# Moved loads, stores and a constants' step in a fused attention and double MoE kernel

## The reference, cut to what matters

```
p_packed = sm_attn(p, k, v)              # 8 batches, 8 heads, 576 tokens, 32 packed rows, head_dim 64
x = sm_attn(q, p_packed, p_packed)       # softmax attention, both times
x = x as (batch, 576, 512)
xk, xr = mu * x + (1 - mu) * x_prev      # two mixes with the token before
k = relu(xk @ w_k) ** 2                  # 512 -> 1024
x = sigmoid(xr @ w_r) * (k @ w_v)        # first MoE part
h = x^T @ U @ V                          # over tokens, rank 32
u = x + h^T
out = u + relu(u @ w_ch1) @ w_ch2        # second MoE part, 512 -> 2048 -> 512
```

## Time and profile before

| | us |
|---|---|
| median of 3 runs | 1382.73 |
| lowest and highest | 1382.36, 1384.01 |
| the profiled execution | 1382.45 |
| its span in the trace | 1380.5 |
| PE busy in the span | 1321.9 |

### The profile page before, as it was taken

The page is one execution under the profiler, slowest core; times in us unless marked ns, Lnnn a source line. Parts: engine busy times, 40 slices in busy tenths (PEclk is TensorE's granted clock), DMA queues, the critical chain, the costliest instruction groups (busy, mean ns, idle before and its releaser), DMA issues.

```text
span 1380.5 us, 21487 instructions
## 1 busy us (share of the span) xinstructions
PE 1321.9 (96%) x7662; PEld 1133.7 (82%) x7662; DVE 958.7 (69%) x1559; ACT 701.4 (51%) x1232; POOL 209.4 (15%) x290
## 2 busy tenths in 40 slices
PE   6799999989998999989999999999999999999997
PEld 5677878878887888878999999888887888788885
DVE  3878878777877876675566765956568575866556
ACT  2456664555555466443545554645355444645352
POOL 5630112222121103422001100200011000200000
PEclk8899999999999999999999999999999999999999
DMA  9645465736465422983888899787666887578755
GB/s 223 146 85 83 130 125 141 149 103 130 123 139 133 99 49 80 282 247 100 261 252 265 249 270 320 238 238 216 199 222 182 260 227 213 182 206 210 219 191 128
DMA packets 439112, 252.50 MB, mean 183 GB/s; under 512 B 314496, under 2 KB 359584, under 8 KB 439008
## 3 DMA queue, kind: packets, MB, share of 16 engines
q1 hardware_dynamic: 432800, 239.25, 64.0%
q0 software_dynamic: 3824, 11.30, 2.7%
q10 hardware_dynamic: 2384, 0.59, 0.2%
HBM read 201.25 MB, written 49.81 MB: 182 GB/s over the span
## 4 chain that ended last, share of the span: by engine, by line
PE 51%; DVE 2%; DMA 1%; issue 1%; SPq 0%; ACT 0%; DVEq 0%; ACTq 0%
PE bank L1144 25%; PE bank L1230 23%; PE bank L887 1%; DMA w_ring<-w_parts 1%; PE bank L1041 1%; PE bank L873 1%; PE bank L852 1%; DVE u_parts L1105 0%; DVE acc L1278 0%; DVE hid_parts L1259 0%; DMA v_stage<-in_moe_V 0%; ACT hid_parts L1253 0%; SPq L1527 0%; DMA x_scratch<-x 0%; PE bank L969 0%
## 5 line engine op out<-in xcount | busy, mean ns | idle before, releaser
L1230 PE MATMUL bank<-hid_parts,w_ring 128*128 128x512 f32 (+1 forms) x1680 | 355.5, 369 | 4.9 <-issue 2.3
L1144 PE MATMUL bank<-u_parts,w_ring 128*128 128x512 f32 (+1 forms) x1680 | 354.0, 368 | 1.0 <-DVE hid_raw L1189 0.8
L1230 PEld LDWEIGHTS bank<-hid_parts,w_ring 128*128 128x128 f32 x1680 | 303.2, 188 | 55.6 <-issue 14.9
L1144 PEld LDWEIGHTS bank<-u_parts,w_ring 128*128 128x128 f32 x1680 | 304.8, 188 | 41.1 <-issue 1.3
L1253 ACT ACTIVATE hid_parts<-hid_raw 128x512 fp32r<-128x512 f32 (+1 forms) x280 | 164.9, 589 | 143.8 <-PE bank L1230 143.2
L1259 DVE TENSOR_TENSOR hid_parts<-hid_raw,hid_parts 128x512 fp32r<-128x512 f32 (+1 forms) x280 | 187.1, 674 | 64.1 <-ACT hid_parts L1253 60.7
L873 PE MATMUL bank<-xk_hi,wk_hi 128*128 128x384 f32 x384 | 132.7, 346 | 0.4 <-DVE x L947 0.4
L873 PE MATMUL bank<-xk_lo,wk_hi 128*128 128x384 f32 x384 | 129.5, 337 | 0.0
L873 PE MATMUL bank<-xk_hi,wk_lo 128*128 128x384 f32 x384 | 129.4, 337 | 0.0
L907 ACT ACTIVATE square<-bank 128x384 f32<-128x384 f32 x96 | 47.0, 489 | 143.9 <-PE bank L873 129.0
L887 PE MATMUL bank<-wv_hi,k_hi 128*128 128x512 f32 x288 | 113.6, 394 | 0.0
(11 more groups left out here) (171 smaller groups left out, 1921.6 us busy)
## 6 DMA issues: line engine op xcount, KB each, us to landing
w_ring<-w_parts SPq DMA_DIRECT2D x560, 256.0 KB, 3.6
w_parts<-early_out SPq DMA_DIRECT2D x21, 896.0 KB, 5.0
w_parts<-piece_out SPq DMA_DIRECT2D x11, 896.0 KB, 4.6
x_scratch<-x SPq DMA_DIRECT2D x144, 64.0 KB, 2.0
kq_parts<-in_k SPq DMA_DIRECT2D x112, 72.0 KB, 2.8
kq_parts<-in_q SPq DMA_DIRECT2D x112, 72.0 KB, 2.4
v_rows<-in_v SPq DMA_DIRECT2D x56, 128.0 KB
x_tiles<-x_scratch SPq DMA_DIRECT2D x6, 1024.0 KB, 6.6
```

The lines of the kernel that those rows point to most:

```text
L1144: last = nc.tensor.matmul(to, wring[:, e % RW, ct, a, :], uc[:, pos, b, ct, 0:w], start=(pos in FRESH and ct == 0 and a == 0 and b == 0), ...
L1230: last = nc.tensor.matmul(role(st, j, BANK_OF[pos])[:, 0:w], wring[:, e % RW, j, a, :], hid[:, no % RH, b, 0:w], start=(pos in FRESH and i ...
```

## The change

- `load_first_v` waits for the first pair of k's heads (`k0_in[0]`) and no longer for the first half of q; the weights' loads behind it still wait for that half.
- `omu` moves behind `norm1`, the last part of the second softmax of batch 0.
- `EARLY_AT` goes from (0, 6, 11, 17, 23, 33, 40) to (0, 5, 10, 15, 23, 30, 36).
- Some attention steps of the FIRST group move by a slot or two.
- The loads of V move from the last chunk to slot 12 of the LAST group, into the upper half of a buffer twice as wide; ACT's split of V also waits for the stores of the pieces of buffer 0. The u steps move one slot later.
- For the last pair, tiles 4 to 7 are stored half by SP and half by ACT.
- Idle turns: 112 for 96 behind `scores2`, 36 for 48 behind `outB`.

```diff
-EARLY, FIRST_AT, EARLY_AT = 18, (23, 31, 38, 45), (0, 6, 11, 17, 23, 33, 40)
+EARLY, FIRST_AT, EARLY_AT = 18, (23, 31, 38, 45), (0, 5, 10, 15, 23, 30, 36)
-IDLE_TURNS = {"first": 24, (0, "scores2"): 96, (0, "outB"): 48}
+IDLE_TURNS = {"first": 24, (0, "scores2"): 112, (0, "outB"): 36}
-        third = batch_slots(15, 17, 19, 20, 21, 22, 23, 25, 26, 28, 30, 34, 36)
-        fourth = batch_slots(37, 38, 40, 41, 42, 43, 44, 45, 47, 49, 50, 53, 55)
+        third = batch_slots(15, 17, 20, 22, 23, 24, 25, 26, 28, 29, 31, 34, 36)
+        fourth = batch_slots(37, 38, 40, 42, 43, 44, 45, 46, 47, 49, 50, 53, 55)
...
+            items += [("b_v_load",)] if s == 12 else []
...
-            items += {0: [("b_loads",)], 3: [("b_v",)], 4: [("u", 0, 0), ("u", 0, 1)], 5: [("u", 0, 2), ("u", 0, 3)],
-                      6: [("u", 0, 4), ("u", 0, 5)], 7: [("u", 0, 6), ("u", 0, 7)], 8: [("b_ring",)],
+            items += {0: [("b_loads",)], 3: [("b_v",)], 5: [("u", 0, 0), ("u", 0, 1)], 6: [("u", 0, 2), ("u", 0, 3)],
+                      7: [("u", 0, 4), ("u", 0, 5)], 8: [("u", 0, 6), ("u", 0, 7), ("b_ring",)],
...
         elif step == "pv":
-            items += [("load_v", 1), ("omu",)]
+            items.append(("load_v", 1))
+        elif step == "norm1":
+            items.append(("omu",))
...
-        v_stage = sb("v_stage", [P, S], scope=early)[:, :]
+        v_stage = sb("v_stage", [P, 2 * S], scope=early)[:, S:2 * S]
...
+    def store_out(eng, p, k, quads=None):
+        nt, half = sum_place(*TILES[k])
+        lo, w = tokens(p, half)
+        eng.wait_ge(turn_ok, len(TILES) * p + k + 1)
+        for quad in quads or (range(2) if shared_out(p, k) else range(4)):
...
+    def shared_out(p, k):
+        return p == NB - 1 and k >= 4
...
+                load_x2(0, 1)
+            elif item[0] == "b_v_load":
+                sp.wait_ge(att.x_act, 2 * B)
+                sp.wait_ge(att.x_dve, 2 * B)
                 for i in range(4):
                     sp.dma_start(v_stage[i * NP:(i + 1) * NP, :], vv).then_inc(v_in, 16)
-                load_x2(0, 1)
...
+        pool.wait_ge(att.k0_in[0], 16 * 2)
+        load_first_v(pool)
         pool.wait_ge(att.q0_in[0], 16 * 4)
-        load_first_v(pool)
...
                 act.wait_ge(v_in, 64)
+                act.wait_ge(piece_stored[0], 16 * len(range(0, PIECES - EARLY, SLOTS_P + 1)))
...
+            elif item[0] == "out" and shared_out(*item[1:]):
+                store_out(act, *item[1:], quads=(2, 3))
```

More of the change, by code:

```diff
@@ L1388, in everything @@
             do_b(item, p)
+    def store_out(eng, p, k, quads=None):
[3 more added lines that the diff above has]
+        for quad in quads or (range(2) if shared_out(p, k) else range(4)):
+            to = out.rearrange("b s d -> (b s) d")[lo:lo + w, nt * P + 32 * quad:nt * P + 32 * quad + 32]
+            eng.dma_start(to.rearrange("(m t) d -> t m d", t=32),
+                          turn_place(p, k)[32 * quad:32 * quad + 32, :].rearrange("t (m d) -> t m d", d=32)
+                          ).then_inc(out_done[min(k, 1)], 16)
+    def shared_out(p, k):
+        return p == NB - 1 and k >= 4
     block = ctx.enter_context(nc.Block())
@@ L1570, in do_b @@
             elif item[0] == "out":
-                p, k = item[1:]
-                nt, half = sum_place(*TILES[k])
-                lo, w = tokens(p, half)
-                no = len(TILES) * p + k
-                sp.wait_ge(turn_ok, no + 1)
-                for quad in range(4):
-                    to = out.rearrange("b s d -> (b s) d")[lo:lo + w, nt * P + 32 * quad:nt * P + 32 * quad + 32]
-                    sp.dma_start(to.rearrange("(m t) d -> t m d", t=32),
-                                 turn_place(p, k)[32 * quad:32 * quad + 32, :].rearrange("t (m d) -> t m d", d=32)
-                                 ).then_inc(out_done[min(k, 1)], 16)
+                store_out(sp, *item[1:])
         everything(sp, first, do_a, do_b)
```

## The result

The changed kernel takes 1360.15 us (median of 4, 1359.69 to 1360.56) beside 1383.37 us for the kernel before on the same chip: a ratio of 0.983 (95% interval 0.980 to 0.985). The forecast was 1354.5 us in a range of 1346 to 1366. The gain was forecast as 28.0 us; from profiled execution to profiled execution it is 21.9 us of span (1380.5 to 1358.6).

A forecast was written before the change was run, and what follows sets the result against it. PE was taken as the bound, busy 1321.9 of 1380.5 us, leaving its idle and low-clock time to win. Terms summed to 30.2 us, less 2.2 kept for small waits: 1382.45 - 28.0 = 1354.5 us, range 1346 to 1366.

The forecast's parts named there:

- The MIDDLE groups: Two MIDDLE groups: piece stores go ahead of v's loads, removing PE's stops and the low clock behind: 5.1 and 6.4 us.
- The last chunk: Last chunk: V loaded from slot 12 removes PE's 4.52 us stop and slow stretch: 7.3 us, bounds 4 and 7.5.
- the end: Last output tiles: two store queues shorten the issue time that paces the end: 3.5 us, bounds 3.0 and 4.0.
- The prologue: Start of the kernel: v earlier, constants' step and idle turns together gain 6.9 us, bounds 3 and 10.
- v earlier: Prologue: loading v sooner lets pv start sooner: 2.0 us taken, bounds 0.5 and 4.9.
- rival 1: Prologue: v's packets hold up q, pv no sooner or 1 to 3 us later; 1358 to 1361, chance 0.15.
- the constants' step: Prologue: `omu` moved away lets DVE's second softmax start 3.4 us sooner, called nearly certain.
- The 112 turns: Prologue: the 16 turns added behind `scores2` lie inside the softmax; without room they would cost up to 2 us.
- The 36 turns: Prologue: 12 fewer turns behind outB let PE start at 55.0 instead of 56.59: 1.5 us, bounds 0.6 and 1.6.
- four issues: LAST group, slot 12: V's load issues cost SP 1.9 us where it waits anyway; no loss in the sum.
- slot 0: Border after the FIRST group: a later store before `e_hi` holds ACT: minus 0.5 us, bounds 0 and minus 4.
- the FIRST slots: FIRST group: steps moved a slot or two remove two PE waits: 1.5 us, bounds 0 and 2.5.

The follow-up runs named there:

- e1: The kernel before with only the new EARLY_AT (0, 5, 10, 15, 23, 30, 36): 1372.13 us, ratio 0.9916 to before.
- e4: The changed kernel with all stores of the last output tiles issued by SP again, one queue: 1362.92 us, ratio 0.9864 to before.
- e12: e9 with 18 of POOL's 24 additions left out (zeros instead, a measurement and no version to use): 1347.09 us, ratio 0.9730 to before.
- e6: The changed kernel with 102 idle turns behind scores2 instead of 112 and 72 behind outB instead of 36: 1358.10 us, ratio 0.9806 to before.
- e2: The changed kernel with V's four loads at slot 31 of the LAST group instead of slot 12: 1355.76 us, ratio 0.9808 to before.
- e8: The kernel before with only V's loads moved to slot 12, with what that needs: 1380.70 us, ratio 0.9971 to before.
- e10: e9 with EARLY_AT starting at slot 1 instead of 0: 1354.77 us, ratio 0.9791 to before.
- e11: e9 with the FIRST group's batch slots as in the kernel before: 1356.09 us, ratio 0.9795 to before.
- e9: The changed kernel with V's loads at slot 31 and 102 and 52 idle turns behind scores2 and outB: 1355.56 us, ratio 0.9798 to before.

## Why the prediction was right, and where it was not

**The MIDDLE groups** (5.1 and 6.4 forecast, 5.5 and 6.6 measured) went by their steps: store ahead of v's loads, ACT's wait gone, PE's stop and its slow stretch gone, and e1 shows that EARLY_AT does it alone. The price of a stop, its length plus 0.45 of the work in the slow stretch, held.

**The last chunk** (7.3 forecast, 6.75 measured) and **the end** (3.5 forecast, 2.5 measured) have the right mechanism. At the end the term was too large: I took 3.0 as the lower bound and kept the transfers behind the last issue at some 2 us; they took 3.5, with both queues' stores landing at once (the DMA share of 1.27). The runs show 2.3 us in the spans and 2.8 in the medians (e4 against after, which were measured in different sessions). The rule of the Trainium skill (DMA: Bandwidth & Descriptors, Issuing engines are not separate DMA queues), that a second issuing engine usually saves little beside the transfer, is right in so far as the transfers took back 1.5 of the 4 us, and too low here with the gain near 1 that I drew from it.

**The prologue** came out at 6.7 for a forecast of 6.9, and that is a coincidence. By its steps:

| place | before | after | shift |
|---|---|---|---|
| pv starts | 22.27 | 22.86 | +0.6 |
| softmax starts | 31.48 | 26.67 | -4.8 |
| softmax ends (norm1) | 46.02 | 37.82 | -8.2 |
| outA starts | 46.08 | 38.87 | -7.2 |
| `mixed` starts | 51.85 | 43.61 | -8.2 |
| `xk_lo` starts | 53.97 | 48.76 | -5.2 |
| first k matmul | 56.59 | 49.86 | -6.7 |

v earlier, 2.0 in the sum, was worth nothing: my rival 1, for which the full queue of the earlier trace rows spoke, and the rule that DMA engines take turns between queues (the Trainium skill, DMA: Bandwidth & Descriptors, Queues, rings and completion order). The trace agrees: v landed in time and q's second half 3.9 us later. The failed step is that I named this evidence as the stronger and still put the term at 2.0, between the bounds, instead of at the 0.5 end. The measured time lies in the 1358 to 1361 that I gave for this rival, and that too is chance: the prologue as a whole came out as forecast, and what is missing was lost elsewhere. The softmax starts 4.8 us sooner: 3.4 by the constants' step, as forecast, and 1.4 because `scores2` starts 0.6 sooner and runs at full clock (1.21 us for 2.18). No run has the constants' step alone; the trace shows DVE's wait for U gone. The softmax itself was 3.4 us shorter, which no edit asked for: in the kernel before, one of its steps took 2.54 us (at 38.71) and one 2.31 (35.71), which in after take 0.62 and 0.82. POOL was adding beside both (34.60 to 37.39 and 38.44 to 41.21), which fits what e12 shows, but it adds beside the softmax in after too. Nothing in the forecast asked for these 3.4 us: as far as it goes, they are luck. `mixed` gave 3.0 of it back. The 112 turns held outA 1.0 us, inside the bound of 2 that I had named. The 36 turns gave their 1.5: the k matmul now follows the start of `xk_lo` by 1.1 us instead of 2.6. But they end 4.4 us ahead of it, and the clock is low behind them: 1.5 us that were not in the sum, for I looked at when `xk_lo` would be ready and not at how long PE would stand if it was late. More turns (e6) kept the clock up here, and it fell at 61.8 us instead.

**Two losses were mis-sized at nothing or nearly so.** For V I wrote that its four issues lie at slot 12, "where it waits anyway". The old trace says otherwise. SP waits 11 us for a piece's buffer ahead of that place, but at the place itself one issue follows the next from 551.13 to 572 us; this is the kernel before, where V's issues were to go in between the two lines:

```profile
552.39 1.11 SPq L1336 DMA_DIRECT2D piece_raw<-in_moe_w_ch  x1
553.55 0.97 SPq L1339 DMA_DIRECT2D piece_raw<-in_moe_w_ch  x1
```

I had taken the queue's wait from its neighbourhood and not looked at its next 20 us. The 2.35 us made the loads behind them 1.6 to 2.4 us later; e2 and e8 show a loss of 2.9 us. At slot 0 I took -0.5 from bounds of 0 and -4; it cost 3.5. Here the size was inside the bounds and the cause was wrong: not ACT behind the store (e10) but DVE, which has no gap there; that the new FIRST slots bring this about rests on e11 and the spread of the traces. My price for the FIRST slots, a gain of 1.5, was right for the group (2.1) and left out the bill behind it.

## What to carry to other kernels

A wait in a queue is free room only if nothing behind it is late already: before a DMA is put into it, follow the next item of that queue to its reader. When an edit shifts work by a slot, look at the stretch behind it for an engine without gaps, not only at the wait that was meant. And when one instruction takes several times what its twins take, look at what the neighbour engine does in the same microseconds before blaming the schedule.

## What the hardware showed that I had not expected

- **DVE beside POOL.** Beside POOL's additions DVE's steps of 0.55 us often took 1.1, and once 8.34. Four steps of `mixed` took 2.21 or 5.27 us by whether POOL paused. Without 18 of 24 additions the kernel is 8.5 us shorter. The Trainium skill (SBUF — State Buffer, Who interferes with whom) says that a DVE instruction with two SBUF inputs contends with a GpSimd instruction that reads SBUF, over a pair of ports that is an exclusive lock. The slower steps fit that. What the runs add is that the wait can be far longer than one instruction: POOL's took about 0.7 us each, so the step of 8.34 us stood behind eleven or so of them, and was not let in between. The long steps of `mixed` did the same behind four additions (after, e9) and behind one (e12); all ended 0.4 us after POOL's last addition. A step with one input of 18 columns took 2.54 us beside such a row in the kernel before; why is open. An arrangement that does the same work elsewhere was not tried.
- **Two queues and q.** q's read slipped by 3.9 us when v's few large transfers ran beside it; v itself came in time for pv.
- **The clock.** It fell after stops of 2.2 us (e1) and 2.7 us (e8) and stayed at 1.00 after stops of 2.1 us (before) and 2.7 us (e11) at the same place. I can't say what decides it.
